# Two gated layers behind retention attention: wide products by seven half-block products, each layer in two stages

## The chip, the core and the metric

The kernel runs on one core of one Trainium2 chip. The metric is the device time of one execution in microseconds (us); the median of three runs stands for a kernel. TensorE (PE in the rows, with PEld for its weight loads) multiplies; VectorE (DVE), ScalarE (ACT) and GpSimd (POOL) do the elementwise work; SyncE (SP) issues the transfers.

## The reference

```python
# attention: B, H, S, D = 4, 8, 576, 64
scores = np.matmul(q, k.transpose(0, 1, 3, 2)) / np.sqrt(D)
ret = scores * Dmat                      # Dmat[i, j] = gamma_h ** (i - j), 0 where j > i
x = np.matmul(ret, v)                    # laid out as 2304 tokens x 512
# first layer: d_model 512, d_ff 1536
xn = x / np.sqrt(np.mean(x * x, axis=-1, keepdims=True) + 1e-06) * rms_g
g = xn @ w_gate
x = (g / (1 + np.exp(-g)) * (xn @ w_val)) @ w_out
# second layer: 512 -> 2048 -> 512
h = x @ w_in
out = np.where(h >= 1, h, np.where(h <= -1, 0.0, (h + 1) ** 2 / 4)) @ w_out2
```

All inputs and the output are float32.

## The kernel before

Every product of the two layers keeps float32 accuracy by splitting each operand a into ah, its rounded part (type fp32r), and al = a - ah, and taking three matmuls: ah x bh, ah x bl and al x bh (`split_products`, L410 to L412). ScalarE or VectorE writes the h part, VectorE or GpSimd subtracts to get the l part.

Attention comes first. It works in 16 head pairs (4 batches of 4): `front` makes the scores (L340), the masked scores on VectorE (`a_r`, L658), the state per chunk (L356, then `a_S`, L672), and `back` the output (L375, L381), which VectorE scales into `a_x` (L684). It is stored to `x_scratch` in memory (DRAM).

Then the 2304 tokens are taken in 6 tiles of 384 (`TOK`), first all through layer one (`body_b`), then all through layer two (`body_c`). The weights are kept on chip as pieces of 128 x 512 (36 in the first layer, 32 in the second), each loaded once through `stage`, rounded (L528) and subtracted (L833). For each of the 12 blocks of 128 features of a tile (f), `gate_val` computes gate and value (4 blocks of K times 3 matmuls each, 384 columns wide), ScalarE takes Silu (L600), VectorE multiplies (L771), ScalarE and VectorE split the product (L591, L759), and `out_b` adds it into four banks of the output at once. Layer two is the same with 16 blocks f, Relu and two VectorE operations for the parabola (L623, L801, L808), and `out_c`, whose matmuls are 512 columns wide. The wide products (gate, value, hidden) are therefore 2880 matmuls of 384 columns, the output of layer one 864 of 384, that of layer two 864 of 512. TensorE's order is the program's: the wide product of f, then the output of f - 1 or f - 2, so that the elementwise work of a block lies beside matmuls. Every engine follows the order written for it, and waits on counting semaphores. The root mean square and the norm of tile t + 1 (L703, L708) and the split of its x (L721, L726, L850) are placed between the blocks of tile t.

## Time and profile before

| | |
|---|---|
| median of 3 runs | 972.72 us (969.67 to 972.99) |
| the profiled execution | 974.46 us, its span 972.6 us |
| PE busy | 940.4 us (97%), 5836 matmuls |
| PEld busy | 890.8 us (92%) |
| DVE busy | 390.4 us (40%), 731 instructions |
| ACT busy | 277.1 us (28%) |
| POOL busy | 117.4 us (12%), 96 instructions |
| moved by DMA | 60.55 MB |
| chain that ended last | PE 90%, DMA 5%, SPq 2%, DVE 1%, issue 1% |

The span runs from the first to the last instruction of the program; the profiled execution's own time is 1.9 us more. Matmuls overlap in the profile, so their mean duration is not what one costs; the distance from one start to the next is.

### The profile page before, as it was taken

The numbers are of one execution on the slowest core, as the hardware profiler recorded it, in microseconds if no ns is written. First come the engines' busy times: TensorE is split into PE (matmuls) and PEld (weight loads), VectorE is DVE, ScalarE is ACT, GpSimd is POOL, SyncE is SP. The second block draws the span as 40 slices with busy tenths as digits, with TensorE's granted clock in tenths as the row PEclk, the third lists the DMA queues.
The fourth block names the chain that finished last, engine by engine and source line by source line (L and its number), as shares of the span: only waits on it lengthen the run. The fifth ranks groups of instructions, "written<-read, shape, count | busy, mean of one in ns | idle before, by whom it ended". The sixth has DMA issues, their size and how long they took to land.

```text
span 972.6 us, 15375 instructions
## 1 busy us (share of the span) xinstructions
PE 940.4 (97%) x5836; PEld 890.8 (92%) x5836; DVE 390.4 (40%) x731; ACT 277.1 (28%) x519; POOL 117.4 (12%) x96
## 2 busy tenths in 40 slices
PE   6887899999999999999999999999999999999997
PEld 5776799999999999999999999899999999998996
DVE  5554733323323322332331164444443544544443
ACT  2323263222122122113124333232222322322322
POOL 1221381100100000010025532000100100100000
PEclk9997999999999999999999999999999999999999
DMA  9999560100010010010034420010100100100000
GB/s 250 290 269 267 161 181 1 45 21 1 12 54 0 0 65 0 0 65 0 0 113 126 131 98 11 1 66 1 37 28 0 65 0 0 65 0 0 33 1 33
DMA packets 28535, 60.55 MB, mean 62 GB/s; under 512 B 3440, under 2 KB 6640, under 8 KB 28496
## 3 DMA queue, kind: packets, MB, share of 16 engines
q1 hardware_dynamic: 28496, 60.02, 20.9%
q8 instruction: 26, 0.43, 0.2%
q14 instruction: 13, 0.11, 0.0%
HBM read 45.85 MB, written 14.16 MB: 62 GB/s over the span
## 4 chain that ended last, share of the span: by engine, by line
PE 90%; DMA 5%; SPq 2%; DVE 1%; issue 1%; ACT 0%; ACTq 0%; DVEq 0%
PE bank L412 29%; PE bank L411 29%; PE bank L410 29%; DMA a_kt<-ktok 4%; PE bank L340 2%; DMA a_q<-qT 1%; SPq L220 1%; PE bank L392 0%; SPq L215 0%; DVE a_r L658 0%; DVE a_S L672 0%; DVE rinv L703 0%; SPq L209 0%; DVE a_x L684 0%; DVE xh L721 0%
## 5 line engine op out<-in xcount | busy, mean ns | idle before, releaser
L410 PE MATMUL bank<-xh,Wh_lo 128*128 128x384 f32 x504 | 169.0, 335 | 1.6 <-DVE xl L726 1.6
L412 PE MATMUL bank<-xh,Wl_lo 128*128 128x384 f32 x504 | 168.9, 335 | 0.0
L411 PE MATMUL bank<-xl,Wh_lo 128*128 128x384 f32 x504 | 168.7, 335 | 0.0
L591 ACT ACTIVATE ah<-ab 128x384 fp32r<-128x384 f32 x168 | 88.4, 526 | 267.5 <-DVE ab L771 145.0
L410 PE MATMUL bank<-xh,Wh_hi 128*128 128x384 f32 x456 | 154.3, 338 | 0.0
L412 PE MATMUL bank<-xh,Wl_hi 128*128 128x384 f32 x456 | 152.9, 335 | 0.0
L411 PE MATMUL bank<-xl,Wh_hi 128*128 128x384 f32 x456 | 152.6, 335 | 0.0
L771 DVE TENSOR_TENSOR ab<-bank,sb 128x384 f32<-128x384 f32 x72 | 40.2, 558 | 271.2 <-PE bank L412 254.5
L759 DVE TENSOR_TENSOR al<-ab,ah 128x384 fp32r<-128x384 f32 x168 | 95.6, 569 | 99.2 <-ACT ah L591 99.2
L801 DVE SCALAR_TENSOR_TENSOR sb<-sb 128x384 f32<-128x384 f32 x96 | 57.9, 603 | 151.1 <-ACT sb L623 151.1
L850 POOL TENSOR_TENSOR xl<-xraw,xh 128x384 fp32r<-128x384 f32 x24 | 30.2, 1257 | 637.9 <-DVE xh L721 637.9
L410 PEld LDWEIGHTS bank<-xh,Wh_lo 128*128 128x128 f32 x504 | 94.6, 188 | 3.9 <-DVE xh L721 1.1
L411 PEld LDWEIGHTS bank<-xl,Wh_lo 128*128 128x128 f32 x504 | 94.6, 188 | 1.8
L623 ACT ACTIVATE sb<-bank,half_s 128x384 f32<-128x384 f32 x96 | 55.6, 579 | 140.1 <-PE bank L412 140.1
L412 PEld LDWEIGHTS bank<-xh,Wl_lo 128*128 128x128 f32 x504 | 94.6, 188 | 0.0
L410 PEld LDWEIGHTS bank<-xh,Wh_hi 128*128 128x128 f32 x456 | 85.6, 188 | 2.5
L411 PEld LDWEIGHTS bank<-xl,Wh_hi 128*128 128x128 f32 x456 | 85.6, 188 | 2.5
L412 PEld LDWEIGHTS bank<-xh,Wl_hi 128*128 128x128 f32 x456 | 85.6, 188 | 0.0
L600 ACT ACTIVATE sb<-bank 128x384 f32<-128x384 f32 x72 | 35.4, 491 | 154.6 <-PE bank L412 154.6
L412 PE MATMUL bank<-Wh_lo,al 128*128 128x512 f32 x162 | 64.1, 396 | 0.0
L411 PE MATMUL bank<-Wl_lo,ah 128*128 128x512 f32 x162 | 64.0, 395 | 0.0
L340 PE MATMUL bank<-a_q,a_k 128*96 128x192 f32 x192 | 41.3, 373 | 22.8 <-DMA a_kt<-ktok 19.2
(64 smaller groups left out, 1383.7 us busy)
## 6 DMA issues: line engine op xcount, KB each, us to landing
stage<-wB SPq DMA_DIRECT2D x36, 256.0 KB, 4.8
stage<-wC SPq DMA_DIRECT2D x32, 256.0 KB, 2.9
a_k<-kT SPq DMA_DIRECT2D x16, 288.0 KB, 6.2
a_q<-qT SPq DMA_DIRECT2D x32, 144.0 KB, 6.0
a_v<-vtok SPq DMA_DIRECT2D x16, 288.0 KB, 7.5
x_scratch<-a_x SPq DMA_DIRECT2D x16, 288.0 KB, 7.8
xraw<-x_scratch SPq DMA_DIRECT2D x6, 768.0 KB, 5.4
y_scratch<-yb SPq DMA_DIRECT2D x6, 768.0 KB, 3.6
```

What stands on the lines that cost most here:

```text
L220: sp.dma_start(a_q[rows, p, h, :, :].rearrange("p c t -> p (c t)"), qT[b, p, rows, :]).then_inc(d_q[p], 16)
L340: mm = pe.matmul(b_sc[g][0:C, (c % 2) * 2 * C:(c % 2 + 1) * 2 * C], a_k[:, i, c * C:(c + 1) * C], a_q[:, p, :, c, :], start=True, stop=True)
L410: pe.matmul(o, wh, mh, start=first, stop=False)
L411: pe.matmul(o, wh, ml, start=False, stop=False)
L412: return pe.matmul(o, wl, mh, start=False, stop=last)
L591: act.activation(ah[:, f % 4, :], ab[:, f % 2, :], ACT.Copy).then_inc(s_ah, 1)
L600: act.activation(sb[:, f % 2, :], b_g[f % 2][:, 0:TOK], ACT.Silu).then_inc(s_s, 1)
L623: act.activation(sb[:, f % 2, :], b_h[f % 4][:, 0:TOK], ACT.Relu, bias=half_s[:, 0:1], scale=0.5).then_inc(s_s, 1)
L759: dve.tensor_tensor(al[:, f % 4, :], ab[:, f % 2, :], ah[:, f % 4, :].bitcast(F32), ALU.subtract).then_inc(s_al, 1)
L771: dve.tensor_tensor(ab[:, f % 2, :], b_v[f % 2][:, 0:TOK], sb[:, f % 2, :], ALU.mult).then_inc(s_a, 1)
L801: dve.scalar_tensor_tensor(out=sb[:, f % 2, :], in0=sb[:, f % 2, :], scalar=1.0, in1=sb[:, f % 2, :], op0=ALU.min, op1=ALU.mult).then_inc( ...
L850: pool.tensor_tensor(xl[:, k, :], xraw[:, k, :], xh[:, k, :].bitcast(F32), ALU.subtract).then_inc(s_xlp, 1)
```

## The change

The wide products are made by seven products of half blocks in place of eight (the Winograd form of Strassen's scheme). A **step** is 256 features of the gate and the value each (layer two: 512 features of hidden) for one tile of 576 tokens: the weights of a **unit** and the tile's x are both cut in halves along K, x also along the tokens (288 each) and the weights along two blocks of features. VectorE makes four sums of the weight blocks of each unit (`unit_sums`, S1 to S4) and four of the x blocks of each tile (`tile_sums`, T1 to T4). Each of the seven products is 12 matmuls of 288 columns, so that a step has 84. There are 24 steps in layer one (12 units, each for two tiles in turn) and 16 in layer two (8 units): `for g in range(GB)` and `for g in range(GB, GALL)`.

The seven products land in four pairs of banks X, Q, Y, R. ScalarE copies X and Q out at four moments (`copy`), VectorE makes the four quarters of the result from copies and banks (`c11`, `c12`, `c22_c21`), and Silu and the gate product, or clamp, parabola and maximum, work on whole results of 1152 or 2304 values per partition.

Each layer is now two stages. In the first the wide products of all steps are made, and the activated product is stored to memory (`a_scratch`, `b_scratch`) and loaded again; in the second the output product is made from it, in chains over all 12 (`chain_y`, 32 chains of 36 matmuls of 288 columns) or 16 blocks (`chain_o`, 18 chains of 48 matmuls of 512 columns). The weights of the wide products are streamed: every unit is loaded (8 transfers of 128 KB, in runs of 512 bytes), summed, rounded by ScalarE (7 operations), and subtracted by GpSimd (7 operations) for its two steps, and in layer one loaded again for the second pair of tiles. The attention result stays on chip (`x_scratch` is gone). All loops over batches and tiles are unrolled. Attention itself is the same work per pair; between its pairs VectorE now also norms tiles 0 and 1, sums and splits them, and sums unit 0.

```diff
-TOK = 384
-NT = NTOK // TOK
+UB, UC = 6, 4
+GB, GC = 2 * 2 * UB, 2 * 2 * UC
+GALL = GB + GC
+NT = 4
+NHT = 2 * NT
+NBLK = NTOK // P
+X, Q, Y, R = range(4)
+INTO = (X, Q, Y, X, Q, X, R)
+FIRST = (True, True, True, False, False, False, True)
+A11, S1, A12, S2, S4, S3, A22 = range(7)
+B11, T1, B21, T2, B22, T3, T4 = range(7)
+T_BY_DVE = (T1, T2, T3, T4)
+B_BY_POOL = (B11, B21, B22)
+HT_SLOT = (2, 0, 1, 2, 0, 1, 0, 1)
...
+            def load_unit(un):
+                i = un % 2
+                for kk, n, dst in ((0, 0, wt[i][:, A11, 1, :, :, :]), (0, 1, a21[i][:, :, :, :]),
+                                   (1, 0, wt[i][:, A12, 1, :, :, :]), (1, 1, wt[i][:, A22, 1, :, :, :])):
+                    for q in range(2):
+                        if un < 2 * UB:
+                            src = wB[3 * (2 * (un % UB) + n) + q]
+                        else:
+                            src = wC[2 * (4 * ((un - 2 * UB) % UC) + 2 * q + n)]
+                        src = src.rearrange("p (j k c) -> p j k c", j=2, k=2)[:, :, kk, :]
+                        sp.dma_start(dst[:, q, :, :], src).then_inc(d_w[i], 16)
...
+            def store_b(g):
+                sp.wait_ge(s_a, g + 1)
+                t = tile_of(g) - NT
+                f = 4 * ((unit_of(g) - 2 * UB) % UC)
+                sp.dma_start(b_s[:, f:f + 4, t * SEQ:(t + 1) * SEQ],
+                             cb[g % 2][:, :, :, :, :].rearrange("p q n h t -> p (q n) (h t)")).then_inc(d_as[g % 2], 16)
...
-            def split_products(o, wpart, xpart, first, last):
-                (wh, wl), (mh, ml) = wpart, xpart
-                pe.matmul(o, wh, mh, start=first, stop=False)
-                pe.matmul(o, wh, ml, start=False, stop=False)
-                return pe.matmul(o, wl, mh, start=False, stop=last)
...
+            def product(g, i):
+                un, T = unit_of(g), tile_of(g)
+                for q in range(2):
+                    o = pair[INTO[i]][:, q, 0:HALF]
+                    for j in range(2):
+                        wh, wl = wc[un % 2][:, i, 0, q, j, :], wc[un % 2][:, i, 1, q, j, :]
+                        xh, xl = xc[T % 2][:, i, 0, j, :], xc[T % 2][:, i, 1, j, :]
+                        pe.matmul(o, wh, xh, start=FIRST[i] and j == 0, stop=False, skip_group_check=True)
+                        pe.matmul(o, wh, xl, start=False, stop=False, skip_group_check=True)
+                        mm = pe.matmul(o, wl, xh, start=False, stop=j == 1, skip_group_check=True)
+                mm.then_inc(s_p, 1)
+            def combined(g, i):
+                un, T = unit_of(g), tile_of(g)
+                if g % 2 == 0:
+                    pe.wait_ge(s_wh, 7 * un + i + 1)
+                    pe.wait_ge(s_wl, 7 * un + i + 1)
+                if fresh_tile(g):
+                    pe.wait_ge(s_xh, 7 * T + i + 1)
+                    if i in T_BY_DVE:
+                        pe.wait_ge(s_xld, 4 * T + T_BY_DVE.index(i) + 1)
+                    else:
+                        pe.wait_ge(s_xlp, 3 * T + B_BY_POOL.index(i) + 1)
+            def step(g):
...
+                combined(g, 3)
+                pe.wait_ge(s_c, 4 * g + 1)
+                product(g, 3)
+                combined(g, 4)
+                pe.wait_ge(s_c, 4 * g + 2)
+                product(g, 4)
+                combined(g, 5)
+                pe.wait_ge(s_c, 4 * g + 3)
+                product(g, 5)
...
+                product(g, 6)
+            for g in range(GB):
+                step(g)
...
+            def copy(g, n):
+                act.wait_ge(s_p, 7 * g + (1, 2, 4, 6)[n])
+                if g:
+                    act.wait_ge(s_d, 4 * (g - 1) + (1, 3, 2, 4)[n])
...
+            def silu(g):
+                act.wait_ge(s_d, 4 * g + 4)
+                t = cb[g % 2][:, 0, :, :, :].rearrange("p n h t -> p (n h t)")
+                act.activation(t, t, ACT.Silu).then_inc(s_f, 1)
...
+            def unit_sums(un):
+                i = un % 2
+                dve.wait_ge(d_w[i], 128 * (un // 2 + 1))
+                def piece(n):
+                    return wt[i][:, n, 1, :, :, :]
+                dve.tensor_tensor(piece(S1), a21[i][:, :, :, :], piece(A22), ALU.add).then_inc(s_S, 1)
+                dve.tensor_tensor(piece(S3), piece(A11), a21[i][:, :, :, :], ALU.subtract).then_inc(s_S, 1)
+                dve.wait_ge(s_S, 4 * un + 1)
+                dve.tensor_tensor(piece(S2), piece(S1), piece(A11), ALU.subtract).then_inc(s_S, 1)
+                dve.wait_ge(s_S, 4 * un + 3)
+                dve.tensor_tensor(piece(S4), piece(A12), piece(S2), ALU.subtract).then_inc(s_S, 1)
+            def tile_sums(T):
+                t, o = tokens(T), xt[T % 2]
...
+                b11, b12, b21, b22 = part(t, 0, 0), part(t, 0, 1), part(t, 1, 0), part(t, 1, 1)
+                dve.tensor_tensor(o[:, T1, 1, :, :], b12, b11, ALU.subtract).then_inc(s_T, 1)
+                dve.tensor_tensor(o[:, T3, 1, :, :], b22, b12, ALU.subtract).then_inc(s_T, 1)
+                dve.wait_ge(s_T, 4 * T + 1)
+                dve.tensor_tensor(o[:, T2, 1, :, :], b22, o[:, T1, 1, :, :], ALU.subtract).then_inc(s_T, 1)
+                dve.wait_ge(s_T, 4 * T + 3)
+                dve.tensor_tensor(o[:, T4, 1, :, :], o[:, T2, 1, :, :], b21, ALU.subtract).then_inc(s_T, 1)
+            def tile_lo(T, i):
+                dve.wait_ge(s_xh, 7 * T + i + 1)
+                if i == T2:
+                    dve.wait_ge(s_T, 4 * T + 4)
+                dve.tensor_tensor(xc[T % 2][:, i, 1, :, :], xt[T % 2][:, i, 1, :, :],
+                                  xc[T % 2][:, i, 0, :, :].bitcast(F32), ALU.subtract).then_inc(s_xld, 1)
...
+            def c11(g):
+                dve.wait_ge(s_p, 7 * g + 3)
+                dve.wait_ge(s_c, 4 * g + 1)
+                if g > 1:
+                    dve.wait_ge(d_as[g % 2], 16 * (g // 2))
...
+                dve.tensor_tensor(cb[g % 2][:, :, 0, 0, :], pair[Y][:, :, 0:HALF], copies[0][:, :, :],
+                                  ALU.add).then_inc(s_d, 1)
+            def c12(g):
+                dve.wait_ge(s_p, 7 * g + 5)
+                dve.wait_ge(s_c, 4 * g + 3)
+                dve.tensor_tensor(cb[g % 2][:, :, 0, 1, :], pair[Q][:, :, 0:HALF], copies[2][:, :, :],
+                                  ALU.add).then_inc(s_d, 1)
+            def c22_c21(g):
+                dve.wait_ge(s_c, 4 * g + 4)
+                dve.tensor_tensor(cb[g % 2][:, :, 1, 1, :], copies[3][:, :, :], copies[1][:, :, :],
+                                  ALU.add).then_inc(s_d, 1)
+                dve.wait_ge(s_p, 7 * g + 7)
+                dve.tensor_tensor(cb[g % 2][:, :, 1, 0, :], copies[3][:, :, :], pair[R][:, :, 0:HALF],
+                                  ALU.subtract).then_inc(s_d, 1)
+            def gated(g):
+                dve.wait_ge(s_f, g + 1)
+                g0, g1 = (cb[g % 2][:, q, :, :, :].rearrange("p n h t -> p (n h t)") for q in range(2))
+                dve.tensor_tensor(g1, g0, g1, ALU.mult).then_inc(s_a, 1)
...
+            def clamp(g):
+                dve.wait_ge(s_d, 4 * g + 4)
+                dve.tensor_scalar(out=cl[:, :, :, :, :].rearrange("p q n h t -> p (q n h t)"),
+                                  in0=cb[g % 2][:, :, :, :, :].rearrange("p q n h t -> p (q n h t)"),
+                                  scalar1=-1.0, scalar2=1.0, op0=ALU.max, op1=ALU.min).then_inc(s_cl, 1)
+            def joined(g, q):
+                dve.wait_ge(s_f, GB + 2 * (g - GB) + q + 1)
+                h = cb[g % 2][:, q, :, :, :].rearrange("p n h t -> p (n h t)")
+                op = dve.tensor_tensor(h, h, cl[:, q, :, :, :].rearrange("p n h t -> p (n h t)"), ALU.max)
+                if q:
+                    op.then_inc(s_a, 1)
...
+            for g in range(GB, GALL):
+                un, n = unit_of(g), g - GB
+                c11(g)
+                if n:
+                    joined(g - 1, 0)
+                with_unit = n % 2 == 0 and un + 1 < 2 * (UB + UC) and n not in (0, 2 * UC) or n in (1, 2 * UC + 1)
+                tile = {0: NT + 1, 2 * UC - 1: NT + 2, 2 * UC: NT + 3}.get(n)
+                if with_unit:
+                    unit_sums(un + 1)
+                if tile:
+                    tile_sums(tile)
+                c12(g)
+                if n:
+                    joined(g - 1, 1)
+                if tile:
+                    tile_lo(tile, T1)
+                c22_c21(g)
+                clamp(g)
+                if tile:
+                    for i in T_BY_DVE[1:]:
+                        tile_lo(tile, i)
+                if g == GALL - 1:
+                    b_lo(0, 0)
+                    b_lo(0, 1)
...
+            def unit_lo(un, i):
+                pool.wait_ge(s_wh, 7 * un + i + 1)
+                if i == 0:
+                    pool.wait_ge(s_S, 4 * un + 4)
+                pool.tensor_tensor(wc[un % 2][:, i, 1, :, :, :], wt[un % 2][:, i, 1, :, :, :],
+                                   wc[un % 2][:, i, 0, :, :, :].bitcast(F32), ALU.subtract).then_inc(s_wl, 1)
...```

Three places of the order of instructions follow. On VectorE, before, in layer two, each block f is three operations (`sb`, `ab`, `al` are the activated block and its split):

```order
L801 SCALAR_TENSOR_TENSOR sb<-sb 128x384
L808 TENSOR_TENSOR ab<-bank,sb 128x384
L759 TENSOR_TENSOR al<-ab,ah 128x384
L721 CAST xh<-xraw 128x384 x3
L726 TENSOR_TENSOR xl<-xraw,xh 128x384
```

The last two rows stand at a tile's end. After, the eighth step of layer two (g = 31) is this, with `cb` the results of the step (67 and 68 are its two buffers), `cl` the clamped copy, `cp` ScalarE's copies, `xt` the sums of tile 6 and `xc` the combined blocks of that tile with both parts:

```order
L1021 TENSOR_TENSOR cb_68<-pair,cp_63 128x2x288
L1109 TENSOR_TENSOR cb_67<-cb_67,cl 128x1152
L981 TENSOR_TENSOR xt_51<-xr_59 128x576
L982 TENSOR_TENSOR xt_51<-xr_59 128x576
L984 TENSOR_TENSOR xt_51<-xr_59,xt_51 128x576
L986 TENSOR_TENSOR xt_51<-xt_51,xr_59 128x576
L1027 TENSOR_TENSOR cb_68<-pair,cp_65 128x2x288
L1109 TENSOR_TENSOR cb_67<-cb_67,cl 128x1152
L992 TENSOR_TENSOR xc_49<-xt_51,xc_49 128x576
L1032 TENSOR_TENSOR cb_68<-cp_66,cp_64 128x2x288
L1035 TENSOR_TENSOR cb_68<-cp_66,pair 128x2x288
L1102 TENSOR_SCALAR cl<-cb_68 128x2304
```

The sums of the tile stand ahead of the second quarter (L1027), and the low part of T1 (L992) behind the second maximum (L1109), in one queue with them. In the steps that load a unit, the four rows L961, L962, L964, L966 of 128x512 stand where the tile's sums stand here.

On GpSimd, before, the whole of layer two has the remaining weight pieces and two operations a tile:

```order
L833 TENSOR_TENSOR Wl_hi<-stage,Wh_hi 128x512 x8
L850 TENSOR_TENSOR xl<-xraw,xh 128x384 x2
```

After, from the unit of steps 26 and 27 to the end (`wc` the weights of a unit, `wq` those of the last output product):

```order
L1168 TENSOR_TENSOR wc_54<-wt_56,wc_54 128x512 x7
L1168 TENSOR_TENSOR wc_53<-wt_55,wc_53 128x512 x7
L1174 TENSOR_TENSOR xc_49<-xr_59,xc_49 128x576 x3
L1174 TENSOR_TENSOR xc_50<-xr_60,xc_50 128x576 x3
L1181 TENSOR_TENSOR wq_93<-wq_r_109,wq_93 128x512
```

Seven subtractions stand there for each unit, three for each tile, and sixteen like the last row.

On ScalarE in layer one, an even step with a unit (copies of banks X, Q, X, X; L741 is Silu, L690 the rounding of the next unit), where before each block had Silu and one copy:

```order
L736 ACTIVATE cp_63<-pair 128x576
L736 ACTIVATE cp_64<-pair 128x576
L741 ACTIVATE cb_68<-cb_68 128x1152
L736 ACTIVATE cp_65<-pair 128x576
L690 ACTIVATE wc_53<-wt_55 128x512 x4
L736 ACTIVATE cp_66<-pair 128x576
L690 ACTIVATE wc_53<-wt_55 128x512 x3
```

The last copy, for which the next step's first product waits, stands behind four roundings; the fourth of these waits for all four sums of the unit.

## Rows read from the trace of the kernel before

**Rows 1.** Stretches: us, PE, PEld, DVE, ACT, POOL busy (count), clock, DMA share, GB/s

```profile
150.00:200.00 50.00, 50.00 (x291) 49.90 (x290) 17.46 (x30) 11.05 (x21) 2.51 (x2) 1.00 0.09 32
700.00:800.00 100.00, 100.00 (x508) 91.10 (x507) 45.09 (x82) 28.91 (x53) 3.08 (x3) 1.00 0.09 31
```

**Rows 2.** The chain that ended last, in order of time (start, us, what)

```profile
113.73 0.41 PE bank L410
...
967.52 0.60 ACT yo L633
```

**Rows 3.** TensorE's timeline (start us, us, instruction), layer one and layer two

```profile
400.00 0.33 PE L410 MATMUL bank<-ah,Wh_hi 128*128 128x384 f32 x1
...
403.99 0.33 PE L412 MATMUL bank<-xh,Wl_hi 128*128 128x384 f32 x1
...
802.33 0.39 PE L410 MATMUL bank<-Wh_lo,ah 128*128 128x512 f32 x1
...
803.95 0.40 PE L411 MATMUL bank<-Wl_lo,ah 128*128 128x512 f32 x1
```

**Rows 4.** Weight loads of TensorE, one group by line (busy us, mean ns)

```profile
L412 PEld LDWEIGHTS bank<-xh,Wl_hi 128*128 128x128 f32 x456 | 85.6, 188 | 0.0
```

**Rows 5.** TensorE's timeline in attention, one head pair

```profile
25.46 2.16 PE L340 MATMUL bank<-a_q,a_k 128*96 128x192 f32 x12 [1.83 <-DMA a_kt<-ktok]
27.55 0.80 PE L356 MATMUL bank<-a_v,a_kd 96*64 96x64 f32 x20
...
29.85 0.34 PE L381 MATMUL bank<-a_q,a_S 128*64 128x96 f32 x4
```

**Rows 6.** VectorE's timeline in attention, one pair (start us, us)

```profile
100.53 1.42 DVE L658 TENSOR_TENSOR a_r<-bank,mask_s 96x384 f32<-96x384 f32 x3
101.87 1.21 DVE L672 SCALAR_TENSOR_TENSOR a_S<-a_S,cdec_s,bank 128x64 f32<-128x64 f32 x4
103.00 0.82 DVE L684 TENSOR_TENSOR a_x<-bank,qdec_s 128x288 f32<-128x288 f32 x2
```

**Rows 7.** Single lines of VectorE and GpSimd: durations ns min/median/max

```profile
L771 DVE TENSOR_TENSOR ab<-bank,sb x72: 556/558/558, 117.7 to 562.2; 128x384 f32<-128x384 f32 x72
...
L759 DVE TENSOR_TENSOR al<-ab,ah x168: 557/558/1641, 118.8 to 963.7; 128x384 fp32r<-128x384 f32 x168
...
L721 DVE CAST xh<-xraw x48: 349/354/1175, 110.7 to 898.6; 128x384 fp32r<-128x384 f32 x48
...
L833 POOL TENSOR_TENSOR Wl_hi<-stage,Wh_hi x32: 1279/1292/1619, 123.1 to 596.6; 128x512 fp32r<-128x512 f32 x32
```

**Rows 8.** Timeline of all engines around 142 us

```profile
140.98 7.86 POOL L833 TENSOR_TENSOR Wl_hi<-stage,Wh_hi 128x512 fp32r<-128x512 f32 x6
...
142.30 1.64 DVE L759 TENSOR_TENSOR al<-ab,ah 128x384 fp32r<-128x384 f32 x1 [0.59 <-ACT ah L591]
```

**Rows 9.** Groups of VectorE and ScalarE by line (busy us, mean ns)

```profile
L703 DVE RECIPROCAL rinv<-rinv 128x192 f32<-128x192 f32 x12 | 16.2, 1346 | 0.0
...
L818 DVE COPY yo<-bank 128x512 f32<-128x512 f32 x6 | 4.1, 692 | 5.7 <-PE bank L412 5.7
...
L528 ACT ACTIVATE Wh_hi<-stage 128x512 fp32r<-128x512 f32 x32 | 19.3, 623 | 8.8 <-DMA stage<-wB 8.7
L600 ACT ACTIVATE sb<-bank 128x384 f32<-128x384 f32 x72 | 35.4, 491 | 154.6 <-PE bank L412 154.6
L633 ACT ACTIVATE yo<-bank 128x512 f32<-128x512 f32 x12 | 6.5, 595 | 23.3 <-PE bank L412 23.3
```

**Rows 10.** Transfers: KB each, median us from issue to landing; SyncE's timeline

```profile
stage<-wC SPq DMA_DIRECT2D x32, 256.0 KB, 2.9
y_scratch<-yb SPq DMA_DIRECT2D x6, 768.0 KB, 3.6
...
4.49 0.43 SPq L209 DMA_DIRECT2D cdec_s<-cdec  x1
4.96 0.43 SPq L209 DMA_DIRECT2D qdec_s<-qdec  x1
```

More of the change, by code:

```diff
@@ new lines, in unit, with tile @@
+            def unit(un):
+                for i in range(7):
+                    unit_lo(un, i)
+            def tile(T):
+                for i in B_BY_POOL:
+                    tile_lo(T, i)
+            tile(0)
+            unit(0)
+            tile(1)
+            for un in range(1, UB + 1):
+                unit(un)
+            tile(2)
+            tile(3)
+            for un in range(UB + 1, 2 * UB - 1):
+                unit(un)
+                if un >= UB + 3:
+                    for f in range(4 * (un - UB - 3), 4 * (un - UB - 2)):
+                        wo_lo(f, 0)
@@ new lines, in _ @@
+            unit(2 * UB - 1)
+            for f in range(8, FB):
+                wo_lo(f, 0)
+            unit(2 * UB)
+            tile(NT)
+            tile(NT + 1)
+            for un in range(2 * UB + 1, 2 * UB + UC + 1):
+                unit(un)
+            tile(NT + 2)
+            tile(NT + 3)
+            unit(2 * UB + UC + 1)
+            unit(2 * UB + UC + 2)
+            for f in range(6):
+                wo_lo(f, 1)
+            unit(2 * UB + 2 * UC - 1)
+            for f in range(6, FC):
+                wo_lo(f, 1)
```

1293 lines of the change are left out of this document (710 added, 583 removed).

## The prediction

> **What bounds the kernel now.** I read the stretches of the span first, to see which engine is never idle. From 150 us on TensorE is busy for the whole of both stretches shown and its granted clock is full, while VectorE stands below half and GpSimd has almost nothing [rows 1]. The chain that ended last agrees: the two layers run from 113.7 us, the last elementwise operation starts at 967.5 us, and nothing but matmuls fills the 853.8 us between [rows 2]. So what counts is the distance between the starts of two matmuls. With 384 columns it is (403.99 - 400.00) / 23 = 0.1735 us, with 512 columns (803.95 - 802.33) / 7 = 0.2314 us [rows 3]. The check: 2880 + 864 = 3744 of the first and 864 of the second are 649.6 + 199.9 = 849.5 us, of 853.8. Before 113.7 us stands attention.
>
> **The change part by part.** I sum the stages on the clock of the span.
>
> *The matmuls.* None in the trace has 288 columns. In proportion to 384 it would be 0.130 us; the line through both distances of [rows 3] gives 0.130 as well, and a fixed part of 0.0135 us over 384 columns at 2.4 GHz gives 0.1335. I take 0.132. The bound at the far end is that a weight load, recorded at 188 ns [rows 4], sets the distance: but starts 0.1735 us apart are closer than that record is long, and in attention 20 loads of 64 columns with their matmuls take 0.80 us, 0.04 each [rows 5], so loads overlap. A step is 84 x 0.132 = 11.1 us and a product 1.58. The wide products then cost 3360 x 0.132 = 444 us in place of 2880 x 0.1735 = 500: a gain of 56. The output of layer one goes from 864 x 0.1735 = 150 to 1152 x 0.132 = 152. The output of layer two stays at 199 or 200. That is all the arithmetic can give, and it is given only while every step has its operands in time.
>
> *Elementwise prices.* VectorE's `ab` (one input in a bank, 384 wide) takes 0.558 us and a copy of 512 takes 0.692 [rows 7, 9], so 1.05 ns an element over about 0.155 us: 576 elements 0.77 us, 512 elements 0.70, 1152 elements 1.37. The clamp of 2304 elements is not in the trace. At that slope it would be 2.6 us; the rounding copy L721, 384 wide from and to on-chip memory, takes 0.35 in place of 0.56 [rows 7], half the slope, which gives 1.35. I take 1.35 since it too has one input tensor, and keep 2.6 for the range. The Trainium skill ("VectorE: DVE Perf Modes", Mode 2×_2P) says that float32 tensor_scalar gets twice the rate because its one tensor uses both read ports; no row here shows a tensor_scalar. ScalarE: 0.62 for a rounding of 512, 0.65 for a copy of 576 from a bank, about 1.1 for 1152 (slope (595 - 491) / 128 ns) [rows 9]. GpSimd: 1.29 for 512 elements [rows 7], an estimated 1.4 for 576. Reciprocal: 1.346 us for 192 [rows 9], so about 4.0 for 576; a norm is this and four operations of some 0.82, 7.3 us.
>
> *VectorE and GpSimd take turns.* `al` (both inputs in on-chip memory) takes 0.558 us, but 1.64 at the worst, while `ab`, with one input in a bank, never leaves 0.558 [rows 7]. The bad one starts at 142.30 in the middle of GpSimd's row of six subtractions [rows 8], and GpSimd's own worst, 1.619, is one VectorE operation's rest longer than its median. So such an operation waits for the end of GpSimd's and GpSimd then for it. In the kernel before GpSimd is busy for 117 us of 973 and this costs nothing. The Trainium skill ("SBUF — State Buffer", the section on the shared port pair) states it as a rule: a VectorE instruction with two SBUF inputs, or in a two-port mode, and a GpSimd one that reads SBUF lock each other out for a whole instruction. By that rule the second layer's wide stage comes to 213 us, without it to 187.
>
> *Gate and value stage, 24 steps, 266 us.* A step has for VectorE `c11`, `c12`, `c21` and `c22` (4 x 0.77) and the gate product 1.37, 4.5 us; a unit's sums add 2.8 every second step, with 9.0 us of GpSimd behind them. All taking turns: 24 x 2.14 + 11 x 2.8 + 2 x 6.2 + 6.6 for the norms and 123 of GpSimd (11 units of 9.0, two tiles of 4.2, twelve weight pieces of 1.29) is 224 us of 266: it fits. In an even step, counted from its start: Silu of the last step ends near 5.1, the gate product 7.1, the sums 9.9, the fourth rounding 10.5, the last copy 11.15, against a step's end at 11.1. So 0.1 to 0.2 us per unit, 2 in all. The unit must be there by 7: eight issues 0.47 apart [rows 10] and a landing of some 2.5 after the last give 5.8. Two places are worse. The norms of tiles 2 and 3 stand in steps 1 and 2 ahead of `c22`: 7.3 us, the second also in turns with GpSimd, so that ScalarE's copy of Q waits for `c22` and product 5 for the copy: 0.7 + 1.6 + 6.4 = 9 us. The sums and low parts of tiles 2 and 3 (8 x 0.77 each, interleaved with 1.29's of GpSimd) in steps 11 and 12 hold up the last copy (3.9), product 2 (1.3) and the next tile's (3): 9 us. With 2 for the output weights: 22. Stage: 288.
>
> *Output of layer one:* 152 + 2 for the first low parts, which start only when the last step is done: 154.
>
> *Second wide stage, 16 steps, 177 us.* Per step 4 x 0.77 + 2 x 1.37 + 1.35 = 7.2 us of VectorE, of which 4.9 in turns with GpSimd. Taking turns: 16 x 4.9 = 78, seven units' sums 20, three tiles 19; GpSimd 7 x 9.0 = 63, three tiles 13, sixteen weight pieces 21. Together 214, less about 14 that may run past the last step: 200 us against 177, so at least 23 of stall. If they did not take turns, VectorE's own 16 x 7.2 + 20 + 19 = 154 us would lie beside 177, and some 10 of stall would be left for the tile steps: 187. A second loop works the same way: `c11` waits until the store of the step two before has landed (1.18 MB; from 3.6 us for 768 KB [rows 10] some 5.1), and from `c11` to the second maximum it is 4.3 us, 7.1 with a unit, plus turns: two steps take about 23.8 in place of 22.2. Followed through, the four ordinary pairs cost 1.6 each, 7 in all; the late unit 13 and tile 5 at the start 7; and tiles 6 and 7 with units 17 and 18 in steps 31 to 36, where product 2 of step 32 waits for a T1 low part that stands behind both maxima, 22. I take 36, stage 213.
>
> *Last output:* 199 + 4: its first chain waits for the low part of the first block of tokens, which VectorE makes behind the last clamp. 203.
>
> *Attention.* TensorE needs 4.6 us per pair, from 25.46 to about 30.05 [rows 5], VectorE 3.3 [rows 6]. The first six pairs go at TensorE's pace, to about 36 us. The other ten are paced by VectorE, at some 4.0, with 34 us between them: two norms (14.6), sums and low parts of tiles 0 and 1 (12.4), sums of unit 0 (2.8), squares added (2 x 2.1), and some 8 lost in turns with GpSimd's thirteen operations there. 36 + 40 + 34 + 8 = 118 us to the first product, in place of 113.7. The lower bound, if TensorE's pace holds and half of the extra hides, is 105; attention's memory traffic is less (no `x_scratch`, one unit in place of 16 pieces), and this was what it waited for.
>
> *Tail:* 4 us, in place of 5.1.
>
> **Sum:** 118 + 288 + 154 + 213 + 203 + 4 = 980 us of span. The profiled execution is 1.9 us over its span and 1.7 over the median, so spans stand for medians here: 980 against 972.7.
>
> **The rivals.**
> 1. *The turns stay off the path (faster).* If VectorE's and GpSimd's operations overlap in most cases, or slack takes them up, the stages are 110, 276, 154, 187, 203 and 4: 934. In between, with half the stalls, 957. For it: TensorE's waits are each with some 5 us of slack (the second product of a step starts at 12.7 us on the clock above and waits for a `c12` that ends at 10.7). Against it: [rows 8], and the two tile steps, where the slack is used up. The stalls that I sum are 22 + 2 + 36 + 4 = 64 us, and attention is 4 later, against 56 gained, less 2 and plus 1 at the tail: with less than 51 of stalls the change is faster.
> 2. *The clamp at 2.6 us.* 16 x 1.25 = 20 more on the engine that sets the pace there: 1000.
> 3. *Unit loads are late.* Runs of 512 bytes are a quarter of any weight piece's. If a unit took 10 us to land, 18 unit steps would stall by 3 each: 1030. The bound from below: 1 MB in 3.8 us of issue is no more than the rates of attention.
> 4. *The distance does not shrink.* If 288 columns still took 0.1735, 4512 x 0.0415 = 187 more: 1165. Two column counts on one line speak against it.
>
> **Numbers.** This measurement can tell about 0.5% from no change, that is 968 to 977.5. My case, all stalls between 52 and 76 (968 to 992), 0.4; rival 1 with what lies between, down to 930, 0.35; rival 2 or more stall than I followed, 992 to 1015, 0.18; rivals 3 and 4, 0.07. Faster 0.35, same 0.15 (all in my case), slower 0.5. The range cuts the lowest and the highest tenth: 944 to 1012. My case's own range is 968 to 992.
>
> **What the profile would show.** Starts 0.132 us apart in chains of 288; the last product before 750 us or after; VectorE's 1152-wide maxima often at 2.4 to 2.7 us, GpSimd's rows at 2 us and more; idle time of TensorE before the first product of step 32 and the second, released by `xc` or `cb` of VectorE; sums of units released by GpSimd's turns and not by `wt` transfers. I am wrong if the maxima stay at 1.37, if TensorE is idle for less than 40 us in both wide stages, or if its waits name transfers.

## The result, and the profile after

| | before | after |
|---|---|---|
| median of 4 runs | 972.86 us (969.67 to 975.73) | 1006.23 us (1003.56 to 1007.9) |
| ratio | | 1.0341, 95% interval 1.0302 to 1.0381 |
| span of the profiled execution | 972.6 us | 1006.1 us |
| mean granted clock of TensorE | 0.993 | 0.959 |

The change makes the kernel 3.4% slower. The forecast was 980 us with slower as the likeliest sign: the sign and the range held, the point is 26 us low. The time lies outside the forecast's main case (968 to 992 us, chance 0.4), in the band from 992 to 1015 that it gave 0.18. The page of the changed kernel begins so (engines, busy time, tenths in 40 slices, the chain that ended last):

```profile
PE 920.4 (91%) x6608; PEld 866.5 (86%) x6608; DVE 548.5 (55%) x652; ACT 397.7 (40%) x604; POOL 309.3 (31%) x196
...
PEclk9978889899989999999999999997899999999999
...
PE 65%; DVE 15%; SPq 7%; DMA 4%; issue 4%; ACT 4%; POOL 1%; ACTq 0%; DVEq 0%
```

TensorE was 97% busy and 90% of the chain; now it is 91% and 65%, and VectorE and SyncE's queue stand in the chain. Cut at the first matmul of each stage (us, PE, PEld, DVE, ACT, POOL busy, clock, DMA share, GB/s), the span reads:

```profile
0.00:124.90 124.90, 90.43 (x1228) 80.00 (x1228) 94.45 (x190) 43.45 (x89) 18.65 (x17) 0.90 0.58 159
124.90:427.00 302.10, 281.55 (x2023) 277.64 (x2020) 176.57 (x194) 150.01 (x230) 137.85 (x95) 0.97 0.33 106
427.00:582.00 155.00, 154.93 (x1151) 154.96 (x1151) 45.48 (x55) 37.74 (x59) 15.38 (x10) 0.99 0.37 122
582.00:803.70 221.70, 194.44 (x1348) 190.05 (x1347) 180.80 (x169) 126.31 (x183) 135.08 (x73) 0.94 0.48 154
803.70:1006.00 202.30, 199.05 (x864) 163.87 (x864) 51.23 (x46) 40.21 (x45) 2.29 (x2) 0.99 0.39 114
```

The five rows are attention, the gate and value stage, the output of layer one, the second wide stage and the last output. Both output stages are full and nearly at full clock (0.99); most of the time is lost in the other three. The waits at the two seams (2.1 and 5.0 us) are moved here to the output that they belong to, as the forecast did:

| stage | forecast | measured | |
|---|---|---|---|
| attention | 118 | 124.9 | +6.9 |
| gate and value, 24 steps | 288 | 300.0 | +12.0 |
| output of layer one | 154 | 157.3 | +3.3 |
| second wide stage, 16 steps | 213 | 216.4 | +3.4 |
| last output | 203 | 203.8 | +0.8 |
| tail | 4 | 3.7 | -0.3 |

TensorE's waits (us in total, times, longest) name ScalarE's copies first:

```profile
PE pair L518 <- ACT cp L736: 26.7, 16, 4.6
PE pair L452 <- DVE a_r L909: 18.4, 4, 7.7
PE pair L465 <- ACT a_kd L660: 6.8, 4, 2.1
...
PE pair L518 <- issue: 4.8, 6, 2.6
...
PE pair L518 <- POOL xc L1174: 3.6, 2, 3.3
PE pair L518 <- DVE xc L992: 3.3, 1, 3.3
PE pair L518 <- POOL wc L1168: 2.8, 1, 2.8
```

ScalarE is only 40% busy, so a late copy is a copy behind something late. VectorE's waits name one such thing:

```profile
DVE wt L961 <- DMA wt<-wC: 14.2, 6, 3.1
DVE cb L1021 <- DMA b_scratch<-cb: 12.9, 9, 2.4
DVE wt L961 <- DMA wt<-wB: 11.0, 8, 5.2
```

These are 25.2 us of waiting for units (`wt`). The forecast expected the sums of a unit to be released by GpSimd's turns "and not by `wt` transfers"; these rows say otherwise. TensorE's own waits in the wide stages name no transfer, and it is idle for 48 us there (302.1 - 281.6 and 221.7 - 194.4), over the 40 that the forecast asked for.

Durations, to set beside [rows 7] (ns min/median/max):

```profile
L1109 DVE TENSOR_TENSOR cb<-cb,cl x32: 1343/1782/2423, 599.8 to 807.0; 128x1152 f32<-128x1152 f32 x32
L1032 DVE TENSOR_TENSOR cb<-cp,cp x40: 743/811/1973, 141.1 to 798.2; 128x576 f32<-128x576 f32 x40
L1102 DVE TENSOR_SCALAR cl<-cb x16: 1359/1672/1814, 595.4 to 800.0; 128x2304 f32<-128x2304 f32 x16
L1168 POOL TENSOR_TENSOR wc<-wt,wc x140: 1263/1297/2432, 78.9 to 781.4; 128x512 fp32r<-128x512 f32 x140
L1021 DVE TENSOR_TENSOR cb<-pair,cp x40: 745/758/760, 131.3 to 793.3; 128x576 f32<-128x576 f32 x40
```

VectorE's operations with both inputs in on-chip memory stretch, and so do GpSimd's; `c11`, with one input in a bank, never does. The clamp (L1102) has one input and stretches too: 1.36 us at the least, 1.67 in the median.

### The profile page after: what moved, and what is told of

Read it like the earlier page. It is cut to its first block, busy times and chain, and to the rows that moved or that the text cites. A ratio compares the mean times of both kernels' runs of the same rounds, so it can differ in the third digit from the quotient of the medians.

```text
span 1006.1 us, 15838 instructions
## 1 busy us (share of the span) xinstructions
PE 920.4 (91%) x6608; PEld 866.5 (86%) x6608; DVE 548.5 (55%) x652; ACT 397.7 (40%) x604; POOL 309.3 (31%) x196
## 4 chain that ended last, share of the span: by engine, by line
PE 65%; DVE 15%; SPq 7%; DMA 4%; issue 4%; ACT 4%; POOL 1%; ACTq 0%; DVEq 0%
PE pair L518 9%; PE pair L520 8%; PE pair L519 8%; PE pair L642 7%; PE pair L644 7%; PE pair L643 7%; SPq L287 6%; PE pair L611 5%; PE pair L613 5%; PE pair L612 5%; PE pair L452 3%; DMA wt<-wC 2%; DMA wt<-wB 2%; DVE cb L1109 2%; DVE xr L949 2%
## 5 line engine op out<-in xcount | busy, mean ns | idle before, releaser
L518 PE MATMUL pair<-xc,wc 128*128 128x288 f32 x1120 | 343.3, 306 | 41.3 <-ACT cp L736 26.7
L519 PE MATMUL pair<-xc,wc 128*128 128x288 f32 x1120 | 338.4, 302 | 0.0
L520 PE MATMUL pair<-xc,wc 128*128 128x288 f32 x1120 | 337.4, 301 | 0.0
L1168 POOL TENSOR_TENSOR wc<-wt,wc 128x512 fp32r<-128x512 f32 x140 | 223.2, 1629 | 344.1 <-DVE wt L966 330.3
L518 PEld LDWEIGHTS pair<-xc,wc 128*128 128x128 f32 x1120 | 218.0, 195 | 48.9 <-ACT cp L736 23.7
L520 PEld LDWEIGHTS pair<-xc,wc 128*128 128x128 f32 x1120 | 218.5, 195 | 0.0
L519 PEld LDWEIGHTS pair<-xc,wc 128*128 128x128 f32 x1120 | 218.4, 195 | 0.1
L736 ACT ACTIVATE cp<-pair 128x576 f32<-128x576 f32 x160 | 103.5, 647 | 196.5 <-PE pair L520 178.0
L642 PE MATMUL pair<-wq,bv 128*128 128x512 f32 x288 | 113.4, 394 | 4.7 <-DVE bv L1116 4.6
L611 PE MATMUL pair<-av,wo 128*128 128x288 f32 x384 | 114.5, 298 | 1.9 <-DVE av L1046 1.9
L612 PE MATMUL pair<-av,wo 128*128 128x288 f32 x384 | 113.9, 297 | 0.0
L613 PE MATMUL pair<-av,wo 128*128 128x288 f32 x384 | 113.5, 296 | 0.0
L644 PE MATMUL pair<-wq,bv 128*128 128x512 f32 x288 | 113.0, 392 | 0.0
L643 PE MATMUL pair<-wq,bv 128*128 128x512 f32 x288 | 113.0, 392 | 0.0
L1116 DVE TENSOR_TENSOR bv<-bv_r,bv 128x1024 fp32r<-128x1024 f32 x36 | 44.9, 1288 | 114.0 <-ACT bv L834 114.0
L690 ACT ACTIVATE wc<-wt 128x512 fp32r<-128x512 f32 x140 | 80.3, 624 | 35.1 <-DMA wt<-wC 11.2
L1021 DVE TENSOR_TENSOR cb<-pair,cp 128x576 f32<-128x576 f32 x40 | 30.3, 757 | 104.7 <-PE pair L520 82.6
L611 PEld LDWEIGHTS pair<-av,wo 128*128 128x128 f32 x384 | 72.6, 189 | 2.1 <-issue 2.1
L613 PEld LDWEIGHTS pair<-av,wo 128*128 128x128 f32 x384 | 72.9, 190 | 0.0
L612 PEld LDWEIGHTS pair<-av,wo 128*128 128x128 f32 x384 | 72.8, 189 | 0.0
L642 PEld LDWEIGHTS pair<-wq,bv 128*128 128x128 f32 x288 | 54.7, 190 | 16.6 <-issue 5.3
```

What stands on the lines that cost most here:

```text
L518: pe.matmul(o, wh, xh, start=FIRST[i] and j == 0, stop=False, skip_group_check=True)
L519: pe.matmul(o, wh, xl, start=False, stop=False, skip_group_check=True)
L520: mm = pe.matmul(o, wl, xh, start=False, stop=j == 1, skip_group_check=True)
L611: pe.matmul(o, wo[f][:, 0, cols], av[i][:, 0, f, :], start=f == 0, stop=False)
L612: pe.matmul(o, wo[f][:, 0, cols], av[i][:, 1, f, :], start=False, stop=False)
L613: mm = pe.matmul(o, wo[f][:, 1, cols], av[i][:, 0, f, :], start=False, stop=f == FB - 1)
```

## What the matmuls do behind a wait

TensorE's timeline of the changed kernel, around the end of step 0 and the start of step 1:

```profile
137.13 0.29 PE L518 MATMUL pair<-xc,wc 128*128 128x288 f32 x1
137.26 0.29 PE L519 MATMUL pair<-xc,wc 128*128 128x288 f32 x1
137.39 0.29 PE L520 MATMUL pair<-xc,wc 128*128 128x288 f32 x1
141.23 0.58 PE L518 MATMUL pair<-xc,wc 128*128 128x288 f32 x1 [3.54 <-ACT cp L736]
141.60 0.44 PE L519 MATMUL pair<-xc,wc 128*128 128x288 f32 x1
141.84 0.44 PE L520 MATMUL pair<-xc,wc 128*128 128x288 f32 x1
142.08 0.44 PE L518 MATMUL pair<-xc,wc 128*128 128x288 f32 x1
```

Two stretches, one ahead of the wait and one behind it (the share behind the counts is the granted clock):

```profile
130.00:137.00 7.00, 7.00 (x55) 7.00 (x54) 0.76 (x1) 1.13 (x2) 0.00 (x0) 1.00 0.59 150
141.30:147.00 5.70, 5.70 (x24) 5.70 (x25) 1.27 (x2) 1.99 (x4) 5.70 (x5) 0.50 0.01 3
```

Ahead of the wait of 3.54 us the starts are 0.133 us apart, behind it 0.24, and it stays so for two products, some 6 us. The granted clock falls from 1.00 to 0.50: the lower of the clock's two levels, 1.2 in place of 2.4 GHz. The same is seen behind all nine waits of 2.6 to 4.6 us in the two wide stages (those at 178.55, 694.6 and 711 us are three of them). Behind the five waits there of 0.8 to 2.1 us the starts stay 0.133 us apart; behind one of 1.9 us at 427.07, ahead of the output of layer one, the clock is at its lower level again, so the length of the wait alone does not decide. The clock's mean fell from 0.993 to 0.959: with only two levels, 2 x 0.041 x 1006 = 82 us at the lower one, in place of 14 before. No term of the forecast had this.

The distances between the starts of the 3360 wide matmuls give the price. Those over 0.3 us are waits: 23 us in the gate and value stage, 26 in the second wide stage. Those of 0.20 to 0.30 us, 192 in all, are matmuls at the lower clock: 8.5 and 11.4 us more than at 0.133. The rest is at 0.133. So in the wide stages 49 us are waits and 20 us are slow matmuls.

## The experiments

Each starts from the changed kernel unless it says otherwise, and "less" means less than its 1006 us. Edits are shown in part; `...` marks what is left out. The kernel before, run on the same chips, had medians of 972.6 to 974.4 us.

**1. GpSimd fills in place of subtracting.** The low parts of the wide weights are left out (zeros): same number of instructions on GpSimd, but none that reads.

```diff
-                pool.tensor_tensor(wc[un % 2][:, i, 1, :, :, :], wt[un % 2][:, i, 1, :, :, :],
-                                   wc[un % 2][:, i, 0, :, :, :].bitcast(F32), ALU.subtract).then_inc(s_wl, 1)
+                pool.memset(wc[un % 2][:, i, 1, :, :, :].bitcast(F32), 0.0).then_inc(s_wl, 1)
```

> The low parts of the unit weights are left out: GpSimd fills them with zeros (140 writes that read nothing) in place of 140 subtractions with two inputs. Theory (VectorE and GpSimd take turns): VectorE's operations with two on-chip inputs fall back to 1.37 us for 1152 wide and 0.77 for 576 wide in the steps with a unit, the second wide stage goes from 217 us to about 195, the first from 300 to about 290, the whole to about 970. Rival (what holds TensorE is the order of VectorE's queue and the late unit loads): the sums still end as late, and the whole stays above 990.

Measured: 975.65 us (ratio to before 1.0019, 0.9976 to 1.0063): 31 us less than the changed kernel. In its trace:

```profile
L1109 DVE TENSOR_TENSOR cb<-cb,cl x32: 1343/1349/1931, 582.0 to 772.2; 128x1152 f32<-128x1152 f32 x32
...
L1168 POOL MEMSET wc<- x140: 517/526/533, 80.0 to 739.5; 128x512 f32 x140
```

The maxima fall from a median of 1.78 to 1.35 us with no change on VectorE. The run also shortens GpSimd's own 140 operations from 1.3 to 0.53 us, so it gives the price of the subtractions as a whole, turns and delay together, and does not part the two. A third of the wide matmuls then multiply by zeros, at the same 0.133 us. In the wide stages the waits fall from 49 to 33 us and the slow matmuls behind them from 20 to 7: nearly half of what is gained there is the clock. The Trainium skill ("SBUF — State Buffer", the section "Who interferes with whom") says that a VectorE operation with two SBUF inputs takes the lock only against a GpSimd operation that reads SBUF; the fill, which only writes and takes 0.517 to 0.533 us in all 140 cases, agrees, and so do the eight maxima that ran beside fills alone, all at 1.35 us.

**2. Units in four transfers of 256 KB.** The host lays the wide weights out a second time so that each piece is one transfer with runs of 2 KB in place of 512 bytes.

```diff
-                    for q in range(2):
...
-                        sp.dma_start(dst[:, q, :, :], src).then_inc(d_w[i], 16)
+                    u = un % UB if un < 2 * UB else UB + (un - 2 * UB) % UC
+                    sp.dma_start(dst.rearrange("p q j c -> p (q j c)"), wU[u, 2 * kk + n]).then_inc(d_w[i], 16)
```

> Each unit is loaded by 4 transfers of 256 KB in runs of 2 KB in place of 8 of 128 KB in runs of 512 bytes; nothing else changes. In the changed kernel the eight issues take 0.61 us each and the last lands 8.3 to 9.5 us after the start of an even step, later than the 7.1 at which VectorE could begin the sums. Theory (late loads cost): units land by 5.5 us, VectorE's 25 us of waiting for wt go to below 3, and the whole to about 990. Rival (turns and queue order are all of it, loads are hidden): within 4 us of 1006.

Measured: 985.35 us (1.0109, 1.0079 to 1.0138), 21 us less, more than expected. SyncE's queue for unit 1, first in the changed kernel, then in this run:

```profile
129.80 1.24 SPq L287 DMA_DIRECT2D wt<-wB  x2
131.08 1.27 SPq L287 DMA_DIRECT2D a<-wB  x2
132.39 2.57 SPq L287 DMA_DIRECT2D wt<-wB  x4
```
```profile
131.72 0.35 SPq L282 DMA_DIRECT2D wt<-wU  x1
132.11 0.43 SPq L282 DMA_DIRECT2D a<-wU  x1
132.59 0.91 SPq L282 DMA_DIRECT2D wt<-wU  x2
```

Eight issues take 5.2 us, 0.64 each; four take 1.8. From the first issue to the first sum it is 7.5 us in the changed kernel (137.26) and 5.4 in this run (137.12). VectorE's wait for units falls from 25.2 to 7.1 us. In the wide stages TensorE's waits fall from 49 to 38 us and its slow matmuls from 20 to 9. The run changes the number of transfers and the length of their runs together and does not say which of the two matters.

**3. The norms of tiles 2 and 3 spread** over steps 1 to 9 (reciprocals in steps 1 and 5, the eight multiplications in 3, 7 and 9), instead of five operations ahead of `c22` in steps 1 and 2.

```diff
-                if g in (1, 2):
-                    norm(g + 1)
...
+                if g in (1, 5):
+                    invert(2 if g == 1 else 3)
+                for b, k in {3: ((2, 0), (2, 1), (2, 2)), 7: ((2, 3), (3, 0), (3, 1)),
+                             9: ((3, 2), (3, 3))}.get(g, ()):
+                    scale(b, k)
```

> The norms of tiles 2 and 3 (a reciprocal of 3.75 us and four operations each) move from steps 1 and 2, ahead of the third quarter, to behind the last quarter of steps 1, 3, 5, 7 and 9, in pieces of at most 3.75 us. Theory (a place in VectorE's queue, with slow clock after it): step 3 goes from 18.9 us to about 12, step 2 unchanged or less, the whole to about 997. Rival (the time is only lent: the same 14 us of VectorE work come back as later copies in the steps where they now stand): above 1003.

Measured: 997.22 us (1.0231, 1.0201 to 1.026), 9 us less, as expected. What it removes, on VectorE in the changed kernel:

```profile
166.65 3.74 DVE L946 RECIPROCAL rinv<-rinv 128x576 f32<-128x576 f32 x1
170.43 6.66 DVE L949 SCALAR_TENSOR_TENSOR xr<-xr,rmsg_s,rinv 128x576 f32<-128x576 f32 x4
177.01 0.74 DVE L1032 TENSOR_TENSOR cb<-cp,cp 128x576 f32<-128x576 f32 x1
```

`c22` (L1032) waits 10.4 us behind the norm, the copy of Q behind it, and TensorE 4.6 us for that copy, until 178.55. The two products behind that wait take 5.9 us, 2.6 of them the slow clock. Over both wide stages the waits are 3 us less in this run (46) and the slow matmuls 7 us less (13).

**4. Tile sums ahead of the first quarter**, and the T1 low part ahead of the second maximum: order alone, the same operations.

```diff
+                if tile:
+                    tile_sums(tile)
                 c11(g)
...
-                if tile:
-                    tile_sums(tile)
```

> In the five steps that prepare a tile, VectorE makes the tile's four sums before the step's first quarter in place of after it, and the low part of T1 before the second maximum. Theory (place in the queue): steps 11 and 12 go from 15.1 and 14.1 us to about 12 each, the four steps from 31 on from 15.6, 17.8, 16.8 and 13.4 to about 13 on average, the whole to about 990. Rival (the steps are bound by the turns with GpSimd and by VectorE's total work, whatever the order): above 1000.

Measured: 1002.32 us (1.0283, 1.0236 to 1.033), 4 us less where 16 were expected: mostly a miss, and on the rival's side (above 1000). Steps 31 to 34 take 15.5, 15.5, 15.6 and 13.6 us in place of 15.6, 17.8, 16.8 and 13.4. VectorE's queue at 683 us of the changed kernel suggests why order helps little there; the four sums are 0.76 us each when GpSimd does nothing (at 89.7 to 92.6):

```profile
683.79 1.84 DVE L981 TENSOR_TENSOR xt<-xr 128x576 f32<-128x576 f32 x1
685.55 1.82 DVE L982 TENSOR_TENSOR xt<-xr 128x576 f32<-128x576 f32 x1
687.30 1.95 DVE L984 TENSOR_TENSOR xt<-xr,xt 128x576 f32<-128x576 f32 x1
689.28 1.87 DVE L986 TENSOR_TENSOR xt<-xt,xr 128x576 f32<-128x576 f32 x1
```

**5. The three together** (2, 3 and 4).

> The changes of the three runs before together: units in four transfers of 2 KB runs, the norms of tiles 2 and 3 spread over steps 1 to 9, and the sums of tiles 2, 3, 6 and 7 ahead of the first quarter. If the stalls are separate, the gains add: 1006 - 21 - 9 - 4 = 972 us. If they are one stock of elementwise work that only moves from place to place, the sum falls short: 980 or more.

Measured: 972.37 us (0.9985, 0.9962 to 1.0008). The gains add (21 + 9 + 4 = 34 us, measured 33.9; the closeness is luck, since each gain is known to 3 to 5 us): these are separate stalls, and with them gone the change is worth nothing either way.

**6. Matmuls that nobody reads, put into four waits.**

```diff
+                for _ in range(FILL.get((g, i), 0)):
+                    pe.matmul(pair[Y if i < 2 else R][:, 0, HALF:512], wc[un % 2][:, n, 0, 0, 0, :], xc[T % 2][:, n, 0, 0, 0:512 - HALF],
+                              start=False, stop=False, skip_group_check=True)
```

> The changed kernel with matmuls whose result nobody reads put into four known waits of TensorE (ahead of step 1, of the fifth product of step 3, of the second products of steps 32 and 33; 118 matmuls of 224 columns in all, in place of 3.8 + 4.9 + 3.7 + 2.9 us of idle time). If the slow clock behind a wait is a cost of its own, the twelve matmuls behind each place are 0.133 us apart again instead of 0.25, the half-clock time falls from 83 to about 70 us and the kernel takes about 998 us. If the waits alone matter and later work would have been late anyway, or fillers push the products back as much as they save: 1004 or more.

Measured: 1008.51 us (1.0352, 1.031 to 1.0394), which by the total speaks for the rival of the expectation. But the trace shows that in three of the four places the fill did not cover the wait; it stood behind it:

```profile
690.75 0.29 PE L521 MATMUL pair<-xc,wc 128*128 128x288 f32 x1
694.88 6.29 PE L529 MATMUL pair<-xc,wc 128*128 128x224 f32 x28 [3.84 <-DVE xc L1008]
```

It waited 3.84 us for the very low part, and then kept TensorE 6.3 us longer. Only the place at step 1 tested the question, so this run decides nothing.

**7. Attention's extra work in smaller portions** (a norm over two pairs, low parts and roundings over two).

```diff
-                if u in (NP + 2, 2 * NP + 2):
-                    norm(u // NP - 1)
-                    tile_sums(u // NP - 1)
+                if u in (NP + 2, 2 * NP + 2):
+                    invert0(u // NP - 1)
+                    scale0(u // NP - 1, (0, 1))
+                if u in (NP + 3, 2 * NP + 3):
+                    scale0(u // NP - 1, (2, 3))
+                    tile_sums(u // NP - 1)
...
```

> The changed kernel with the extra work of attention in smaller portions: a norm over two pairs, the low parts of a tile over two, the roundings of a tile and of unit 0 over two, none behind another. If attention is late because long portions hold the pair behind them, the first product comes at about 118 instead of 124.9 and the kernel takes about 1000 us. If VectorE's total in attention is the limit, the first product stays within 2 us of 124.9 and the kernel within 3 of 1006.

Measured: 1000.3 us (1.0276, 1.0223 to 1.0328), the first wide product at 118.9 in place of 124.9. The portion it breaks up, in the changed kernel:

```profile
79.05 3.74 DVE L946 RECIPROCAL rinv<-rinv 128x576 f32<-128x576 f32 x1
82.83 6.82 DVE L949 SCALAR_TENSOR_TENSOR xr<-xr,rmsg_s,rinv 128x576 f32<-128x576 f32 x4
...
92.49 1.48 DVE L909 TENSOR_TENSOR a_r<-pair,mask_s 96x384 f32<-96x384 f32 x3
```

13.4 us lie between two pairs. TensorE's waits for `a_r` fall from 18.4 to 8.1 us in all, those for `a_kd` rise from 6.8 to 11.8.

**8. All four rearrangements** (2, 3, 4 and 7).

> All four rearrangements together. If the gains add, about 966 us, which would be below the 973 of the kernel before. If they draw on the same stock: 975 to 985.

Measured: 966.25 us (0.9916, 0.989 to 0.9943). This version leaves nothing out, and it takes 0.8% less than the kernel before. Mean clock 0.982; stages 117.0, 280.5, 155.2, 209.4 and, with the tail, 202.4.

**9. Fills again, where they cover the wait:** ahead of the wait for blocks and weights in steps 32 and 33, and in steps 1, 21, 29 and 37, with 17 to 30 matmuls each.

```diff
+                fill(g, 1, FILL_EARLY)
                 combined(g, 1)
```

> Again unread matmuls of 224 columns in waits of TensorE of the changed kernel, now ahead of the wait for weights and blocks where that is the long one: 30 ahead of step 1, 17 ahead of step 21, 28 of step 29, 25 of step 37, 30 ahead of the second product of step 32 and 23 ahead of that of step 33. In the run before, the place at step 1 had its two products behind it in 3.3 us instead of 5.9 with the wait unchanged; the other three stood behind the wait they were to cover. If the clock is a cost of its own: two to three us less at steps 1, 32 and 33 and one at 29, half-clock time at 60 us or less, and 996 to 999 us. If the time is taken again by the next elementwise result: 1004 or more.

Measured: 998.21 us (1.0272, 1.0218 to 1.0326), 8 us less, as the theory of the clock has it. The place shown above, now:

```profile
136.13 0.29 PE L522 MATMUL pair<-xc,wc 128*128 128x288 f32 x1
136.27 3.50 PE L530 MATMUL pair<-xc,wc 128*128 128x224 f32 x30
139.83 0.40 PE L520 MATMUL pair<-xc,wc 128*128 128x288 f32 x1
140.07 0.30 PE L521 MATMUL pair<-xc,wc 128*128 128x288 f32 x1
140.20 0.29 PE L522 MATMUL pair<-xc,wc 128*128 128x288 f32 x1
```

The gap is as long as before (3.70 us in place of 3.84), but the starts behind it are 0.133 us apart: step 1 takes 11.3 us in place of 13.9. At steps 29, 32 and 33 the first two products behind the gap take 3.2 to 3.4 us in place of 4.8 to 5.9. The clock's mean is 0.978. In the wide stages the waits are 3 us longer in all (52 in place of 49) and the slow matmuls 11 us less (9 in place of 20), which is the 8 us gained. So the slow clock is a cost of its own, 1.6 to 2.6 us behind each of these four waits. The place at step 21 had a wait of 2.1 us with no slow matmuls behind it, and gains nothing.

**10. All four, and the fill of run 1** (again without the low parts of the wide weights).

> The four rearrangements with GpSimd's 140 weight subtractions replaced by fills with zeros (leaves out the low parts of the wide weights). If what is left above the matmuls is turns between VectorE and GpSimd, the wide stages come to about 271 and 188 us (268.6 and 179 are the matmuls alone) and the kernel to 930 to 940. If it is VectorE's own work and the order of its queue: 955 or more.

Measured: 946.79 us (0.9735, 0.9687 to 0.9783), between the two expectations: stages 118.8, 274.7, 153.7, 195.2. The gate and value stage loses nothing more after step 0 (11.2 to 11.3 us a step); the second wide stage still has steps 32, 33 and 36 at 15.2, 13.6 and 14.7. GpSimd's subtractions are worth another 19 us, most of it in the second wide stage.

**11. Copy first:** in run 8, the last copy of a step ahead of the next unit's roundings.

```diff
-                if with_unit:
-                    for i in range(4):
-                        unit_hi(un + 1, i)
...
                 copy(g, 3)
                 if with_unit:
-                    for i in range(4, 7):
+                    for i in range(7):
                         unit_hi(un + 1, i)
```

> The four rearrangements, and on ScalarE the last copy of a step ahead of the seven roundings of the next unit, where three or four of these stood before it. In the run of the four, ten of TensorE's waits, 9.8 us in all, end with a copy. If the roundings are what holds the copies, these waits fall below 5 us and the kernel takes about 962 us. If the copies are late by the copies' own inputs, or the roundings, now later, hold GpSimd and the next step's first copy as long: 965 to 969, no difference to the run of the four.

Measured: 968.02 us (0.9951, 0.993 to 0.9972): no gain. TensorE's waits for copies fall from 9.8 to 3.9 us, but waits for the roundings themselves rise:

```profile
PE pair L513 <- ACT wc L685: 5.2, 3, 2.2
PE pair L513 <- ACT cp L728: 3.9, 4, 1.3
```

In run 8 the first of these was 0.9 us. The wait was moved, not removed.

## Why the forecast was right or wrong, step by step

- **The matmuls: right.** 288 columns take 0.133 us (forecast 0.132), an undisturbed step 11.2 us (11.1). The output stages are within 3.3 and 0.8 us.
- **The turns: right in kind, and with what hangs on them the largest single cost.** Run 1 took away 31 us, the clock's part among them. Rival 1 (934) is out. In size the forecast was high: it had the 1152-wide maxima at 1.37 and often at "2.4 to 2.7"; the median is 1.78 us, and one of 32 is over 2.3. The second wide stage took 216.4 us against 213 with turns and 187 without, and that closeness is luck: the forecast had 36 us of waits there and no slow matmuls, the trace has 26 and 11.
- **The clamp: right.** 1.36 us alone, the choice of 1.35, and 1.67 in the median in turns with GpSimd; the 2.6 of rival 2 is out. Alone it is 0.59 ns an element against 1.17 of the maxima, and so the trace agrees with the Trainium skill ("VectorE: DVE Perf Modes", Mode 2×_2P), by which a float32 tensor_scalar gets twice the rate.
- **The norms: right in path, the size partly luck.** 9 us summed, 9 measured by run 3, in the path described (`c22`, copy of Q, the fifth product of step 3). But the forecast's 9 were all waits, with 6.4 at the longest; the longest is 4.6, and 2.6 more come from the slow matmuls behind it.
- **Tiles 2 and 3: right in size.** Steps 11 to 14 take 15.1, 14.1, 12.3 and 12.7 us, 9.4 more than four undisturbed ones, against 9 (the forecast's own terms, 3.9, 1.3 and 3, add up to 8.2). Steps 31 to 36 give 23 against the 22 for tiles 6 and 7. Both measured figures hold slow matmuls that the forecast did not have. Run 4 shows that the reason given, that a low part stands behind both maxima, is worth little. That the amount of work in turns binds instead is argued and only in part shown: without the subtractions (run 1) steps 11 and 31 take 11.8 and 11.3 us, but step 32 still takes 17.9.
- **Units: wrong.** "The unit must be there by 7: eight issues 0.47 apart [rows 10] and a landing of some 2.5 after the last give 5.8." The rows of the kernel before [rows 10] are of transfers with long runs; these issues take 0.64 us each. In the first wide stage VectorE stands idle for the unit at most even steps and begins its sums 7.4 to 9.0 us into the step; in step 0 it is 12.3, because the first issue waits until 129.80 for the products that sum the squares. In run 2 the sums of most of these steps begin at 6.9. What was priced at 2 us in the first wide stage and at a part of 14 in the second (7 for the ordinary pairs, 7 for unit 13 with tile 5) brought 21 us when the loads were made faster (run 2). It is rival 3 in kind, at less than its 50 us.
- **The slow clock: missing.** The forecast costed a wait at its own length. Behind the nine waits of 2.6 to 4.6 us in the wide stages the next two products mostly took 4.8 to 5.9 us where 3.2 would do, 20 us in all by the distances between starts. That alone is most of the 26 by which the point was low. Run 9 recovers 8 us in six places. The runs that remove waits recover it with them: 13 us of the clock in run 1, 11 in run 2, 7 in run 3, by the same count. On the other side, the waits in the wide stages were priced too high: 22 + 36 = 58 us, measured 49.
- **Attention: mis-sized, 118 for 124.9.** The forecast added up the work and left out that it comes in portions, 13.4 us between two pairs, in which TensorE runs dry and then slow (its clock is 0.90 over this stage, and no run parts the two). Spread out (run 7), it takes 118.9.

As a whole: the arithmetic gave its 56 us, and the stalls took more. The forecast's own test was that the change is faster with less than 51 us of stalls beside 4 in attention. That limit left out the 4.3 us which the kernel before lost between its matmuls; by the forecast's own stages it is 972.7 - (980 - 64) = 56.7 us. The measured stalls are over both. What stands above the 444, 152 and 199 us of matmuls is 300.0 - 266 + 216.4 - 177 + 157.3 - 152 + 203.8 - 199 = 83.5 us, and attention is 11.2 later. Against it stand 54.5 us less of matmuls (849.5 - 795), the 4.3 that the kernel before lost between its own, and 1.4 at the tail: 34.5 us more, where the spans differ by 33.5. With the stalls of runs 2, 3, 4 and 7 gone, the same arithmetic wins 0.8%.

## What to carry to other kernels

Saving multiplications by adding elementwise work pays only while each step's elementwise chain, with its transfers, fits beside the matmuls. Count VectorE's two-input operations, and one like the clamp here, as one queue with GpSimd's subtractions where both read on-chip memory. Price a transfer by its own shape: issues of short runs cost more, and where a sum has no slack, as in the unit steps here, the time that they add ahead of it reaches the matmuls. Price a stall of TensorE at its length and, where it is as long as the 2.6 to 4.6 us of this case, at the slower matmuls behind it as well (1.6 to 2.6 us each here). When several waits are separate, as these were, they can be removed one by one, and the gains add. When a stage's total comes out as forecast, look at its parts: here two errors met.
